# Strassen's seven products for the first matmul of a second MLP layer, over pairs of token chunks, on one Trainium2 core

## The chip, the cores and the metric

The kernel runs on one core of one Trainium2 chip. The metric is the device time of one execution in microseconds (us), median of three. Engines: PE (TensorE), DVE (VectorE), ACT (ScalarE), POOL (GpSimd) and SP, whose queue issues all the DMAs.

## What is computed

Attention over pooled keys and values, and two MLP layers behind it, all in float32:

```python
q, k, v: [8, 8, 576, 64]      # pool = 8, Sp = 72
k_p = k.reshape(B, H, Sp, pool, D).mean(axis=3)
v_p = v.reshape(B, H, Sp, pool, D).mean(axis=3)
scores = scale * np.matmul(q, k_p.transpose(0, 1, 3, 2))
...                            # softmax, times v_p
x = np.ascontiguousarray(attn_out.transpose(0, 2, 1, 3)).reshape(B * S, H * D)   # [4608, 512]
h = np.maximum(x @ w_in, 0.0)         # layer 1, w_in [512, 2048]
y = h * h @ w_out                     # w_out [2048, 512]
h = y @ w_in2                         # layer 2, same shapes
g = np.where(h >= 1, h, np.where(h <= -1, 0.0, (h + 1) ** 2 / 4.0))
out = g @ w_out2
```

## The kernel before

The 4608 tokens are cut into NC = 9 chunks of 512. Layer 1 takes chunks 0 to 8, layer 2 chunks 9 to 17 (c counts through, so NC = 9 is the first chunk of layer 2). d_ff = 2048 is cut into NF = 16 blocks f of 128, d_model = 512 into four blocks.

Every float32 product is made of three fp32r matmuls, on the high and the low part of each operand: high x high, high x low, low x high. `w_hi` and `w_lo` hold both parts of w_in (columns 0 to 511 of each block) and w_out (columns 512 to 1023).

A chunk on PE (`chunk`, L990): for every f, `output(c, f)` (L967; four columns m of the output, three matmuls each, into the four banks of `ps_y`, L985) and then `hidden(f + 2)` (L936; four k blocks by three matmuls into bank f % 2 of `ps_h`, L944), for the last two f of the next chunk. Each is 12 matmuls of 128x128 by 128x512.

Between them an activation makes `g_hl`, two buffers of g's high and low part. Layer 1 (`hidden1`): ACT's relu (L574) and square (L576), DVE's square (L734) and low part (L738). Layer 2 (`hidden2`): DVE clips h (L745), ACT squares (L581), DVE takes the maximum with h (L748), ACT casts the high part (L584), DVE subtracts for the low part (L751).

At a chunk's end layer 1 splits the output once more (`take_y`: ACT L592, DVE L758) and stores both parts to DRAM (`store_y`, L343), from where `load_y` (L313) fetches them as layer 2's operand. Layer 2 copies its output (`take_out`, DVE L765) and stores it (`store_out`, L350). A column of `ps_y` is free for the next chunk once it is taken (`y_taken`).

All queues are written out by hand and served in order: `chunk` on ACT and DVE has the order of the activations, the attention slots of the next batch (chunks 0 to 7 only) and, in chunk NC - 1, the splits of layer 2's weights (L510, L663). SP in the chunks about the change: `store_y(NC-3)`, four `load_x` (L305) for chunk NC - 1, `store_y(NC-2)`, the loads of layer 2's weights, `store_y(NC-1)`, then four `load_y` and a `store_out` for each chunk of layer 2.

## Time and profile before

| | |
|---|---|
| median of 3 runs | 1763.51 us (1763.29 to 1766.1) |
| the profiled execution's own time | 1764.07 us |
| its span, first to last instruction | 1762.3 us |
| PE busy | 1747.7 us (99%) |
| DVE, ACT, POOL busy | 760.3, 552.0, 226.6 us |
| mean granted clock of PE | 0.999 |

PE's busy time counts modelled ends of overlapping matmuls, so it says that PE hardly ever stands still, not that it does the least work it could. Starts of instructions are a sounder measure of its pace than durations. The slices of the page are 44 us each; layer 2 takes the last 18 of the 40.

### The profile page before, as it was taken

What the parts mean: (1) busy time and instruction counts of PE and PEld (TensorE: products, weight loads), DVE (VectorE), ACT (ScalarE), POOL (GpSimd) and SP (SyncE); (2) the same over time, 40 slices, a digit from 0 to 9 for tenths busy, and PEclk for the clock granted to TensorE, in tenths of its full rate; (3) what the DMA queues carried; (4) which work ended last, traced back from release to release, by engine and by line L of the source; (5) the groups of instructions that cost most, each with busy time, mean ns of one, the idle gap of its engine ahead of it and who ended that gap; (6) DMA issues with size and microseconds to landing.
All of it is one profiled execution on the core that took longest, in us unless ns stands there. A gap on an engine that the chain in (4) does not pass through costs nothing.

```text
span 1762.3 us, 22444 instructions
## 1 busy us (share of the span) xinstructions
PE 1747.7 (99%) x8374; PEld 1411.7 (80%) x8374; DVE 760.3 (43%) x1207; ACT 552.0 (31%) x973; POOL 226.6 (13%) x254
## 2 busy tenths in 40 slices
PE   9999999999999999999999999999999999999999
PEld 7777777777777777778888788888888888888887
DVE  6654434444343444443235434343434343434343
ACT  5443333333333333332234322222222222222222
POOL 5422313133131331310000000000000000000000
PEclk9999999999999999999999999999999999999999
DMA  6544233142421424222044202020202020202000
GB/s 167 142 134 130 75 117 86 55 132 74 129 73 61 125 74 132 78 66 96 0 138 149 96 0 72 1 71 0 71 0 71 0 71 0 71 0 71 0 25 24
DMA packets 117072, 126.95 MB, mean 72 GB/s; under 512 B 40192, under 2 KB 72448, under 8 KB 116992
## 3 DMA queue, kind: packets, MB, share of 16 engines
q1 hardware_dynamic: 116992, 125.86, 23.2%
q8 instruction: 53, 0.87, 0.2%
q14 instruction: 27, 0.22, 0.0%
HBM read 80.74 MB, written 45.09 MB: 71 GB/s over the span
## 4 chain that ended last, share of the span: by engine, by line
PE 97%; DVE 2%; issue 0%; ACT 0%; POOL 0%; ACTq 0%; POOLq 0%
PE ps_h L944 44%; PE ps_y L985 44%; PE ps_a L894 2%; PE ps_a L918 2%; PE ps_a L931 2%; PE ps_a L908 1%; DVE sq_f L734 1%; PE ps_y L826 0%; PE ps_a L843 0%; DVE probs L674 0%; PE ps_y L864 0%; ACT act_f L574 0%; DVE stat L672 0%; PE ps_y L875 0%; PE ps_h L854 0%
## 5 line engine op out<-in xcount | busy, mean ns | idle before, releaser
L944 PE MATMUL ps_h<-xc,w_hi 128*128 128x512 f32 x2288 | 715.2, 394 | 0.0
L944 PEld LDWEIGHTS ps_h<-xc,w_hi 128*128 128x128 f32 x2288 | 423.0, 188 | 93.6 <-issue 9.2
L944 PE MATMUL ps_h<-xc,w_lo 128*128 128x512 f32 x1144 | 446.8, 391 | 0.2 <-issue 0.2
L985 PE MATMUL ps_y<-w_hi,g_hl 128*128 128x512 f32 x1152 | 379.4, 390 | 3.1 <-DVE stage L758 2.2
L985 PE MATMUL ps_y<-g_hl,w_hi 128*128 128x512 f32 x1152 | 366.2, 399 | 0.4 <-DVE g_hl L738 0.4
L734 DVE TENSOR_TENSOR sq_f<-act_f 128x512 f32<-128x512 f32 x144 | 111.5, 774 | 408.5 <-ACT act_f L574 402.9
L985 PEld LDWEIGHTS ps_y<-w_hi,g_hl 128*128 128x128 f32 x1152 | 216.9, 188 | 49.1 <-DVE stage L758 2.6
L985 PEld LDWEIGHTS ps_y<-g_hl,w_hi 128*128 128x128 f32 x1152 | 209.6, 188 | 56.2 <-issue 16.3
L581 ACT ACTIVATE act_f<-act_f,half_bias 128x512 f32<-128x512 f32 x144 | 104.1, 723 | 480.1 <-DVE act_f L745 480.1
L944 PEld LDWEIGHTS ps_h<-xc,w_lo 128*128 128x128 f32 x1144 | 214.9, 188 | 47.4 <-issue 0.8
L985 PE MATMUL ps_y<-g_hl,w_lo 128*128 128x512 f32 x576 | 225.7, 392 | 0.0
L985 PE MATMUL ps_y<-w_lo,g_hl 128*128 128x512 f32 x576 | 224.8, 390 | 0.0
L745 DVE TENSOR_SCALAR act_f<-ps_h 128x512 f32<-128x512 f32 x144 | 99.5, 691 | 251.9 <-PE ps_h L944 251.9
L574 ACT ACTIVATE act_f<-ps_h 128x512 f32<-128x512 f32 x144 | 86.0, 598 | 361.3 <-PE ps_h L944 360.5
L748 DVE TENSOR_TENSOR act_f<-ps_h,act_f 128x512 f32<-128x512 f32 x144 | 99.6, 691 | 113.8 <-ACT act_f L581 113.8
L751 DVE TENSOR_TENSOR g_hl<-act_f,g_hl 128x512 fp32r<-128x512 f32 x144 | 99.7, 693 | 98.8 <-ACT g_hl L584 98.8
L450 POOL TENSOR_TENSOR kv_raw<-kv_raw 72x512 f32<-72x512 f32 x112 | 120.5, 1076 | 115.8 <-DMA kv_raw<-in_k 111.4
L985 PEld LDWEIGHTS ps_y<-g_hl,w_lo 128*128 128x128 f32 x576 | 108.1, 188 | 24.5
L985 PEld LDWEIGHTS ps_y<-w_lo,g_hl 128*128 128x128 f32 x576 | 108.5, 188 | 22.4
L584 ACT CAST g_hl<-act_f 128x512 fp32r<-128x512 f32 x144 | 89.3, 620 | 109.1 <-DVE act_f L748 109.1
L738 DVE TENSOR_TENSOR g_hl<-sq_f,g_hl 128x512 fp32r<-128x512 f32 x144 | 109.8, 762 | 7.9 <-DVE sq_f L734 2.4
L467 POOL TENSOR_TENSOR probs<-probs,stat 96x432 f32<-96x432 f32 x56 | 53.5, 955 | 386.8 <-DVE stat L689 386.8
(81 smaller groups left out, 931.2 us busy)
## 6 DMA issues: line engine op xcount, KB each, us to landing
mlp_out_hl<-stage SPq DMA_DIRECT2D x36, 512.0 KB, 4.4
xc<-mlp_out_hl SPq DMA_DIRECT2D x36, 512.0 KB, 5.9
xc<-attn_out_hl SPq DMA_DIRECT2D x32, 512.0 KB, 4.0
attn_out_hl<-xo_hl SPq DMA_DIRECT2D x56, 288.0 KB, 2.3
out<-stage SPq DMA_DIRECT2D x36, 256.0 KB, 2.1
stage<-in_moe_w_in SPq DMA_DIRECT2D x32, 256.0 KB, 3.6
stage<-in_moe_w_out SPq DMA_DIRECT2D x32, 256.0 KB, 4.3
kv_raw<-in_k SPq DMA_DIRECT2D x28, 288.0 KB
```

The costliest lines, as they stand in the source:

```text
L450: nc.gpsimd.tensor_tensor(raw[:, :, 0:width], raw[:, :, 0:width], raw[:, :, width:2 * width], ALU.add).then_inc(kv_add, 1)
L467: nc.gpsimd.tensor_tensor(groups(probs[:, u % 2, :]), groups(probs[:, u % 2, :]), row_stat(u % 2, 3), ALU.mult).then_inc(probs_ready, 1)
L574: nc.scalar.activation(act_f[:, f % 2, :], ps_h[:, f % 2, :], ACT.Relu).then_inc(relu_done, 1)
L581: nc.scalar.activation(act_f[:, f % 2, :], act_f[:, f % 2, :], ACT.Square, bias=half_bias[:, 0:1], scale=0.5).then_inc(ramp_done, 1)
L584: nc.scalar.copy(g_hl[:, f % 2, 0, :], act_f[:, f % 2, :]).then_inc(g_hi_done, 1)
L734: nc.vector.tensor_tensor(sq_f[:, f % 2, :], act_f[:, f % 2, :], act_f[:, f % 2, :], ALU.mult).then_inc(square_done, 1)
L738: nc.vector.tensor_tensor(g_hl[:, f % 2, 1, :], sq_f[:, f % 2, :], g_hl[:, f % 2, 0, :].bitcast(F32), ALU.subtract).then_inc(g_ready, 1)
L745: nc.vector.tensor_scalar(act_f[:, f % 2, :], ps_h[:, f % 2, :], 1.0, -1.0, ALU.min, ALU.max).then_inc(clip_done, 1)
L748: nc.vector.tensor_tensor(act_f[:, f % 2, :], ps_h[:, f % 2, :], act_f[:, f % 2, :], ALU.max).then_inc(bend_done, 1)
L751: nc.vector.tensor_tensor(g_hl[:, f % 2, 1, :], act_f[:, f % 2, :], g_hl[:, f % 2, 0, :].bitcast(F32), ALU.subtract).then_inc(g_ready, 1)
L944: mm = nc.tensor.matmul(ps_h[:, f % 2, :], left[:, f, kd * P:(kd + 1) * P], xc[:, buf, right, kd, :], start=(kd == 0 and n == 0), stop=(kd ...
L985: mm = nc.tensor.matmul(ps_y[:, m, :], left, right, start=(f == 0 and n == 0), stop=(f == NF - 1 and n == 2))
```

## The change

Layer 2's first product is made for two chunks a and b at once, for chunks 1 to 8 of the nine (pair p is chunks NC+1+2p and NC+2+2p); chunk NC stays as it was. A product of 2 x 2 blocks (tokens of a or b, two halves of d_model, two blocks f) takes 7 products by Strassen's scheme (in Winograd's form), with sums and differences of the operands, where it took 8.

- The sums of w_in and their high and low parts are made once, in chunk NC - 2 (`split_wq` on ACT and DVE, SP's `load_wq` and `store_wq`), stored to DRAM (`wq`, 1.8 MB for each of the 8 block pairs), and fetched in layer 2 one block pair at a time into `xc` (`load_wp`).
- `store_y` stores layer 1's output of chunks 1 to 8 once, in float32, without a split; `take_y` is then ACT's copy alone. `load_raw` fetches a pair's tokens; `diff`, `op_high` and `op_low` make the 7 operands of 2 blocks each in the space of w_in.
- PE, phase a: in step s it makes the outputs of chunk a for blocks 2s and 2s+1, and between their columns the 7 products of block pair s + 1, in the order of `STEP`. The products cycle through four banks, `ps_a` and `ps_h`. The activation's inputs are sums of products, made by DVE (`combine`); ACT adds 1, cuts at 0 and squares (`ramp`), DVE clips and takes the maximum (`bend`). Chunk a's g goes to `g_hl` at once, chunk b's stays on chip in float32 (`g_late`, tile `late(f)`).
- PE, phase b: the outputs of chunk b from `late(f)`, high part by ACT (`g_high`), low part by DVE (`g_low`). Meanwhile ACT and DVE make the next pair's operands (`HIGH_AT`, `LOW_AT`, `DIFF_AT`), and in the last step PE makes the next pair's first 7 products.
- On SP the first two attention chunks are taken out of the loop, as chunk 0's output is still stored in two parts. POOL sets one more constant.

The diff, cut to its core (empty lines left out):

```diff
+    NP = NF // 2
+    NPAIR = (NC - 1) // 2
+    PRODUCTS = [(0, 0), (4, 2), (1, 3), (5, 5), (2, 4), (3, 1), (6, 6)]
...
+    STEP = [(None, 0), (0, 0), (None, 1), (0, 1), (None, 2), (0, 2), (None, 3), (0, 3), (None, 4), (1, 0), (None, 5),
+            (1, 1), (1, 2), (1, 3), (None, 6)]
...
+    DIFF_AT = {4: [(T1, 0), (T1, 1), (T2, 0)], 5: [(T2, 1)], 7: [(T4, 0), (T4, 1)], 8: [(T3, 0), (T3, 1)]}
+    HIGH_AT = {4: SPLITS[0:2], 5: SPLITS[2:5], 6: SPLITS[5:8], 8: SPLITS[8:10], 9: SPLITS[10:12], 10: SPLITS[12:14]}
+    LOW_AT = {5: SPLITS[0:2], 6: SPLITS[2:5], 7: SPLITS[5:6], 8: SPLITS[6:7], 9: SPLITS[7:10], 10: SPLITS[10:13],
+              11: SPLITS[13:14]}
...
+                    if c.at(0):
+                        sp.dma_start(ys_v[m, :, :, bass.ds(c.times(CHUNK), CHUNK)],
+                                     stage[:, m, :].rearrange("p (l t) -> p l t", l=2)
+                                     ).then_inc(y_stored[m], DMA)
+                    else:
+                        sp.dma_start(ys_v[m, :, 0, bass.ds(c.times(CHUNK), CHUNK)], stage[:, m, 0:CHUNK]
+                                     ).then_inc(y_stored[m], DMA)
...
+                if n >= 2:
+                    sp.wait_ge(wq_ready, 3 * (n - 1))
+                sp.dma_start(wq_raw[:, n % 2], w_in2.rearrange("(k p) (f c) -> f p k c", p=P, c=2 * P)[n]
+                             ).then_inc(wq_loaded[n % 2], DMA)
...
+            def load_wp(n):
+                sp.dma_start(pieces(n % 2 * NPROD, NPROD).bitcast(F32), wq[n]).then_inc(wp_loaded[n % 2], DMA)
...
+                for s in range(NP - 2):
+                    sp.wait_ge(product_done, p.times(NP * NPROD, NPROD * (s + 1)))
+                    load_wp(s + 2)
+                if more:
+                    sp.wait_ge(product_done, p.times(NP * NPROD, NPROD * (NP - 1)))
+                    load_wp(0)
+                    sp.wait_ge(product_done, p.times(NP * NPROD, NPROD * NP))
+                    load_raw(False, p.plus(1))
+                store_out(a)
+                if more:
+                    sp.wait_ge(op_ready, p.times(2 * NPROD, 4 * NPROD))
+                    load_wp(1)
+                store_out(a.plus(1))
...
+            load_wq(0)
+            load_wq(1)
+            for n in range(NP):
+                store_wq(n)
+                if n + 2 < NP:
+                    load_wq(n + 2)
...
+            for half in range(2):
+                sp.wait_ge(wq_stored[half], DMA * NP)
+            load_raw(True, At(0))
...
+            sp.wait_ge(h_ready, NC * NF)
+            load_wp(0)
+            sp.wait_ge(h_ready, (NC + 1) * NF)
+            load_wp(1)
+            store_out(At(NC))
+            with sp.Fori(0, NPAIR - 1) as i:
+                pair(At(0, i, 1), At(NC + 1, i, 2), True)
+            pair(At(NPAIR - 1), At(2 * NC - 2), False)
...
+                    if c.at(0):
+                        nc.scalar.copy(stage[:, m, 0:CHUNK].bitcast(F32R), ps_y[:, m, :]).then_inc(y_hi_done, 1)
+                    else:
                         act.wait_ge(y_stored[m], c.times(DMA))
-                    nc.scalar.copy(stage[:, m, 0:CHUNK].bitcast(F32R), ps_y[:, m, :]).then_inc(y_hi_done, 1)
+                        nc.scalar.copy(stage[:, m, 0:CHUNK], ps_y[:, m, :]).then_inc(y_taken, 1)
...
+                if part == 0:
+                    act.wait_ge(wq_loaded[n % 2], DMA * (n // 2 + 1))
...
+                    nc.scalar.copy(wq_hl[:, 0:2, 0], wq_raw[:, n % 2, :, 0:P].rearrange("p (o j) c -> p o j c", o=2)
+                                   ).then_inc(wq_hi_done, 1)
+                    nc.scalar.copy(wq_hl[:, 2, 0], wq_raw[:, n % 2, 2:4, P:2 * P]).then_inc(wq_hi_done, 1)
+                else:
+                    act.wait_ge(wq_sum_done, 4 * (n + 1))
...
+                nc.scalar.copy(w_hi[:, n, 0:DM], split_input(first, o, j)).then_inc(op_hi_done, 1)
...
+                act.wait_ge(y_step, c.times(YS, f - 1 if f >= 2 else -YS + NF - 1 if f == 0 else 0))
+                nc.scalar.copy(g_hl[:, f % 2, 0, :], source).then_inc(g_hi_done, 1)
+            def ramp(g, n, tile, h, at):
+                act.wait_ge(sum_ready, g.times(NPROD, at))
+                nc.scalar.activation(tile, h, ACT.Relu, bias=one_bias[:, 0:1]).then_inc(pair_relu, 1)
+                act.wait_ge(pair_relu, g.times(4, n))
+                nc.scalar.activation(tile, tile, ACT.Square, scale=0.5).then_inc(pair_ramp, 1)
...
+            def pair_step(a, g, fp):
+                act.wait_ge(product_done, g.times(NPROD, 1))
...
+                nc.scalar.copy(p1_copy, pair_bank[NPROD * fp % 4]).then_inc(p1_copied, 1)
+                ramp(g, 1, act_f[:, 0, :], p1_copy, 2)
+                act.wait_ge(pair_bend, g.times(4, 1))
+                g_high(a, 2 * fp, act_f[:, 0, :])
+                ramp(g, 2, act_f[:, 1, :], h21, 4)
+                ramp(g, 3, late(2 * fp + 1), u3, 5)
+                act.wait_ge(pair_bend, g.times(4, 2))
+                g_high(a, 2 * fp + 1, act_f[:, 1, :])
+                ramp(g, 4, late(2 * fp), u2, 7)
+            def pair(p, a, more):
+                b = a.plus(1)
+                for s in range(NP - 1):
+                    pair_step(a, p.times_at(NP, s + 1), s + 1)
+                for f in range(NF):
+                    act.wait_ge(pair_bend, p.times(4 * NP, 4 * (f // 2 + 1)))
+                    g_high(b, f, late(f))
+                    if more:
+                        for o, j in HIGH_AT.get(f, []):
+                            op_high(False, p.plus(1), o, j)
+                if more:
...
+                    if c.at(NC - 2):
+                        split_wq(f // 2, f % 2)
+                    if c.at(NC):
+                        for o, j in HIGH_AT.get(f - 2, []):
...
+            def split_wq(n, part):
...
+                if part == 0:
...
+                    nc.vector.tensor_tensor(wq_sum[:, 0], a21, a22, ALU.add).then_inc(wq_sum_done, 1)
+                    nc.vector.tensor_tensor(wq_sum[:, 2], a11, a21, ALU.subtract).then_inc(wq_sum_done, 1)
...
+                    nc.vector.tensor_tensor(wq_sum[:, 1], wq_sum[:, 0], a11, ALU.subtract).then_inc(wq_sum_done, 1)
...
+                    nc.vector.tensor_tensor(wq_sum[:, 3], a12, wq_sum[:, 1], ALU.subtract).then_inc(wq_sum_done, 1)
+                else:
...
+                nc.vector.tensor_tensor(diff_tile[o, j], left, right, ALU.subtract).then_inc(diff_done, 1)
...
+                nc.vector.tensor_tensor(w_lo[:, n, 0:DM], split_input(first, o, j), w_hi[:, n, 0:DM].bitcast(F32),
...
+            def g_low(c, f, source):
...
+                nc.vector.tensor_tensor(g_hl[:, f % 2, 1, :], source, g_hl[:, f % 2, 0, :].bitcast(F32),
...
+            def bend(g, n, tile, h):
...
+                nc.vector.scalar_tensor_tensor(tile, tile, 1.0, h, ALU.min, ALU.max).then_inc(pair_bend, 1)
...
+                dve.wait_ge(p1_copied, g.times(1, 1))
...
+                combine(1, u2, p6, p1_copy)
+                dve.wait_ge(sum_ready, g.times(NPROD, 1))
+                combine(2, p1_copy, p2, p1_copy)
+                combine(3, u3, p7, u2)
+                bend(g, 1, t11, p1_copy)
+                g_low(a, 2 * fp, t11)
+                dve.wait_ge(sum_ready, g.times(NPROD, 3))
+                combine(4, h21, u3, p4, ALU.subtract)
+                dve.wait_ge(sum_ready, g.times(NPROD, 4))
+                combine(5, u3, p5, u3)
+                combine(5, u2, p5, u2)
+                bend(g, 2, t21, h21)
+                bend(g, 3, t22, u3)
+                if taking is not None:
+                    take_out(taking)
+                g_low(a, 2 * fp + 1, t21)
+                dve.wait_ge(sum_ready, g.times(NPROD, 6))
+                combine(6, u2, p3, u2)
+                bend(g, 4, t12, u2)
...
+                for f in range(NF):
+                    g_low(b, f, late(f))
+                    if f == 0:
+                        take_out(a)
+                    if more:
+                        pair_ops(False, p.plus(1), f)
+                if more:
+                    pair_step(b.plus(1), p.times_at(NP, NP), 0, b)
+                else:
+                    take_out(b)
...
+                    if c.at(NC - 2):
+                        split_wq(f // 2, f % 2)
+                    if c.at(NC):
+                        pair_ops(True, At(0), f - 2)
...
+            pair_step(At(NC + 1), At(0), 0, At(NC))
...
-                for m in range(MT):
+                if 0 in columns:
+                    pe.wait_ge(g_ready, c.times(NF, f + 1))
+                for m in columns:
...
+            def product(p, g, fp, n):
...
+                if n == 0:
+                    pe.wait_ge(wp_loaded[fp % 2], p.times(DMA * NP // 2, DMA * (fp // 2 + 1)))
+                    if fp == 0:
+                        pe.wait_ge(op_ready, p.times(2 * NPROD, 2 * NPROD))
+                if n < 4 and not g.at(0):
+                    pe.wait_ge(sum_ready, g.times(NPROD, (3, 4, 6, 7)[n] - NPROD))
+                if n == 3 and g.at(0):
+                    pe.wait_ge(g_ready, (NC + 1) * NF)
+                if n == 4:
+                    pe.wait_ge(p1_copied, g.times(1, 1))
+                if n > 4:
+                    pe.wait_ge(sum_ready, g.times(NPROD, n - 4))
+                weights = piece(fp % 2 * NPROD + left)
+                for j in range(2):
+                    hi, lo = weights[:, j * P:(j + 1) * P], weights[:, (2 + j) * P:(3 + j) * P]
+                    for i, (lhs, rhs) in enumerate(((hi, w_hi), (hi, w_lo), (lo, w_hi))):
+                        mm = nc.tensor.matmul(bank, lhs, rhs[:, 2 * right + j, 0:DM],
+                                              start=(j == 0 and i == 0),
+                                              stop=(j == 1 and i == 2))
+                mm.then_inc(product_done, 1)
+            def pair_step(c, f, p=None, g=None, fp=None):
+                for of, n in STEP:
+                    if of is not None:
+                        output(c, f + of, 2, [n])
+                    elif g is not None:
+                        product(p, g, fp, n)
...
+                for s in range(NP):
+                    if s + 1 < NP:
+                        pair_step(a, 2 * s, p, p.times_at(NP, s + 1), s + 1)
+                    else:
+                        pair_step(a, 2 * s)
+                for s in range(NP):
+                    if s + 1 == NP and more:
+                        pair_step(b, 2 * s, p.plus(1), p.times_at(NP, NP), 0)
+                    else:
+                        pair_step(b, 2 * s)
...
+                for f in range(NF if layer == 1 else NF - 2):
...
+            chunk(At(NC), 1, False, 2)
+            pair_step(At(NC), NF - 2, At(0), At(0), 0)
+            with pe.Fori(0, NPAIR - 1) as i:
+                pair(At(0, i, 1), At(NC + 1, i, 2), True)
+            pair(At(NPAIR - 1), At(2 * NC - 2), False)
```

## Rows read from the trace of the kernel before

**Rows 1.** The page: busy time by engine, and the granted clock in 40 slices.

```profile
PE 1747.7 (99%) x8374; PEld 1411.7 (80%) x8374; DVE 760.3 (43%) x1207; ACT 552.0 (31%) x973; POOL 226.6 (13%) x254
...
PEclk9999999999999999999999999999999999999999
```

**Rows 2.** The page: the chain that ended last, by engine.

```profile
PE 97%; DVE 2%; issue 0%; ACT 0%; POOL 0%; ACTq 0%; POOLq 0%
```

**Rows 3.** PE's waits from 800 to 1762 us: in total, times, longest.

```profile
PE ps_y L985 <- DVE stage L758: 2.2, 1, 2.2
PE ps_y L985 <- DVE g_hl L751: 0.9, 1, 0.9
```

**Rows 4.** Timeline of PE: start, length (us), operation, [idle before].

```profile
1202.72 0.39 PE L985 MATMUL ps_y<-w_hi,g_hl 128*128 128x512 f32 x1
...
1205.44 0.61 PE L944 MATMUL ps_h<-xc,w_hi 128*128 128x512 f32 x2
```

**Rows 5.** Timeline of DVE: one block's chain, and the next clip.

```profile
1202.92 0.69 DVE L745 TENSOR_SCALAR act_f<-ps_h 128x512 f32<-128x512 f32 x1 [1.89 <-PE ps_h L944]
...
1205.77 0.69 DVE L751 TENSOR_TENSOR g_hl<-act_f,g_hl 128x512 fp32r<-128x512 f32 x1 [0.69 <-ACT g_hl L584]
1208.36 0.69 DVE L745 TENSOR_SCALAR act_f<-ps_h 128x512 f32<-128x512 f32 x1 [1.89 <-PE ps_h L944]
```

**Rows 6.** Groups by line: count, busy us, mean ns, idle before with releasers.

```profile
L581 ACT ACTIVATE act_f<-act_f,half_bias 128x512 f32<-128x512 f32 x144 | 104.1, 723 | 480.1 <-DVE act_f L745 480.1
...
L584 ACT CAST g_hl<-act_f 128x512 fp32r<-128x512 f32 x144 | 89.3, 620 | 109.1 <-DVE act_f L748 109.1
...
L748 DVE TENSOR_TENSOR act_f<-ps_h,act_f 128x512 f32<-128x512 f32 x144 | 99.6, 691 | 113.8 <-ACT act_f L581 113.8
...
L734 DVE TENSOR_TENSOR sq_f<-act_f 128x512 f32<-128x512 f32 x144 | 111.5, 774 | 408.5 <-ACT act_f L574 402.9 <-issue 5.6
...
L679 DVE TENSOR_TENSOR xo_hl<-ps_a,xo_hl 128x288 fp32r<-128x288 f32 x56 | 25.2, 451 | 32.4 <-ACT xo_hl L565 32.4
...
L674 DVE TENSOR_TENSOR probs<-ps_a,stat 96x432 f32<-96x432 f32 x56 | 33.8, 603 | 1.9
```

**Rows 7.** Timeline where a layer-2 chunk begins: first output block, the copies.

```profile
1153.76 0.39 PE L985 MATMUL ps_y<-w_hi,g_hl 128*128 128x512 f32 x1
...
1156.48 0.61 PE L944 MATMUL ps_h<-xc,w_hi 128*128 128x512 f32 x2
...
1151.98 2.48 DVE L765 COPY stage<-ps_y 128x512 f32<-128x512 f32 x4
```

**Rows 8.** L985's instructions: what its idle time waited for, us and times.

```profile
  issue: 16.3, 37
```

**Rows 9.** Start of chunk NC - 2: SP's issues, PE's first output; windows.

```profile
798.99 3.09 SPq L343 DMA_DIRECT2D mlp_out_hl<-stage  x4
802.20 3.70 SPq L305 DMA_DIRECT2D xc<-attn_out_hl  x4
...
801.54 0.62 PE L985 MATMUL ps_y<-g_hl,w_hi 128*128 128x512 f32 x2
...
800.00:812.00 12.00, 12.00 (x55) 9.94 (x54) 3.52 (x6) 2.46 (x4) 0.00 (x0) 1.00 0.99 345
896.00:902.00 6.00, 6.00 (x28) 4.95 (x28) 1.67 (x3) 1.23 (x2) 0.00 (x0) 1.00 0.93 291
```

**Rows 10.** Layer 2's start: timeline, and a window (us, busy by engine, PEclk, DMA share, GB/s).

```profile
976.58 2.06 ACT L592 CAST stage<-ps_y 128x512 fp32r<-128x512 f32 x4 [1.47 <-DVE w_lo L663]
...
977.95 0.19 PEld L985 LDWEIGHTS ps_y<-w_hi,g_hl 128*128 128x128 f32 x1 [2.59 <-DVE stage L758]
...
981.99 0.59 PEld L944 LDWEIGHTS ps_h<-xc,w_hi 128*128 128x128 f32 x2
...
980.00:982.00 2.00, 2.00 (x7) 1.52 (x6) 0.97 (x2) 0.93 (x2) 0.00 (x0) 0.50 1.03 381
```

**Rows 11.** Timeline at the tail: the last output block.

```profile
1755.96 0.50 PE L985 MATMUL ps_y<-w_hi,g_hl 128*128 128x512 f32 x1 [0.93 <-DVE g_hl L751]
```

204 lines of the change are left out of this document (166 added, 38 removed).

## The prediction

> **What bounds the kernel now.** The page comes first: TensorE (PE) is busy 99% of the span, VectorE 43%, ScalarE 31%, and the granted clock reads 9 in every slice [rows 1]. The chain of waits gives PE 97% of the span [rows 2]. The list of waits, cut to the part after attention, then shows how little PE lacks: it waits twice, 2.2 us for layer 2's first output columns and 0.9 us for the last block of g [rows 3]. So time is the number of TensorE slots times the slot, and the question is whether the slots taken out stay out.
>
> The slot is read from two starts on the timeline: the 12 matmuls of an output block run from 1202.72 to 1205.44 [rows 4], 2.72 us, 0.227 us each. The same block's clip starts 5.44 us apart [rows 5], which is 24 slots. The printed matmul durations (0.39) overlap and are of no use for this.
>
> **What the change removes.** Per pair of chunks and per pair of blocks f, the first product took 2 x 2 x 12 = 48 matmuls; now it takes 7 products of 2 (j) x 3 (hi/lo passes) = 42. With 8 block pairs and 4 chunk pairs that is 6 x 32 = 192 slots. The output matmuls stay as they were. 192 x 0.2267 = 43.5 us. The new matmuls have the same operand shapes as the old, so I give them the same slot.
>
> **Phase a (chunk a, products of the next block pair).** A step has 42 + 24 = 66 slots, 14.96 us. In STEP, the products end at 1.36, 3.40, 5.44, 7.48, 9.52, 11.56 and 14.96, an output column (0.68 us) between them. Durations: ScalarE's activation 0.72 [rows 6], which I give both halves of a ramp, a cast 0.62 [rows 6]; VectorE's add or subtract 0.69 [rows 6], and from 0.69 to 0.77 for scalar_tensor_tensor, which the trace doesn't have (L734, the dearest of this size, is 0.77); I take 0.69, as L748 is the nearest form. A dependent instruction on VectorE starts 0.03 later (1.9 us over 56 of L674). VectorE has 7 sums, 4 bends and 2 splits: 13 x 0.72 = 9.4 us of 14.96. ScalarE has 1 copy, 8 ramp halves and 2 casts: 7.6 us. Both fit.
> Then order. Both engines are served in order, so I walk the step; a bank can be read 0.2 us after its last slot's end, as the clip at 1202.92 follows the block that ends at 1202.72 [rows 4, 5]. Third sum at 7.7, first bend 9.1, g of the even block ready at 10.5, wanted by PE at 16.3 (next step, after product 0). Fourth sum 11.2, both fifth sums 13.1, bends to 14.8, odd block's g 15.5, wanted at 24.5. Last sum 16.2, last bend 18.4; the next step's first sum wants that tile free at 18.6. The banks come free at 7.7 (wanted 14.96), 11.2 (17.0), 13.1 (19.0), 16.2 (21.1); the copy of product 0 is made by 18.3 (23.1). The smallest PE slack is some 5 us. Where chunk b of the last pair is taken out in the same step, VectorE has four copies more, 2.48 us [rows 7]: the last sum moves to 18.8 (21.1), still 2.3 us in hand. I charge nothing; without this cover each us costs 1 us in each of 32 steps.
>
> **More waits.** Some 10 waits stand in a step of 66 slots. The row for this is the chunk boundary: the output block with four column waits runs from 1153.76 to 1156.48 [rows 7], 2.72 us again, so a met wait costs nothing. From above, the trace books 16.3 us of idle on 37 weight loads of L985 [rows 8]: 0.44 each over 320 waits is 141 us, and 0.14 each eats the gain. The boundary is the nearer case: 0.
>
> **From a to b.** Formerly a block of the first product covered take_out; now output(b, 0) follows output(a, 15). With output(a, 15) ending at 5.44 after the last step, the column copies (0.60 apart) end at 5.0, 5.7, 6.4, 7.1; they are wanted at 5.44, 6.12, 6.80, 7.48. The next g is ready at 7.8, wanted at 8.16. That is 0.4 us in hand: 0, at most 4 x 1 us.
>
> **Phase b (chunk b's outputs from g kept on chip).** PE takes 2.72 us a block, and between blocks 4 and 11 VectorE has 8 splits of g and 22 operations for the next pair, up to four a block. Back to back (0.60 apart, as the four copies) 2.4 us; each dependent on the one before, 2.9. g's chain (cast, then split: 1.4 us after output f-2) leaves 1.2 us in hand, and 7 blocks x 0.2 = 1.3 uses it up: 0 to 0.3 us at each of three places. I take 0.5 in all; the upper bound is below. Chunk NC carries the same 22 operations inside the old scheme: the chain takes 3.54 us (1202.92 to 1206.46), leaving 1.89 idle [rows 5], and three operations at 0.60 take 1.8. Here g is ready 1.7 us before PE wants it (1206.46; its output block starts 5.44 after 1202.72, at 1208.16): nothing.
>
> **Transfers.** A step needs 1.8 MB of weight sums. The engines moved 345 GB/s over 12 us [rows 9], so 5.3 us of 14.96, issued a whole step ahead. Storing the sums in chunk NC-2 moves 2.3 MB in 10.9 us (two blocks), 215 GB/s. Hidden. load_y in layer 2 goes, load_raw (2.1 MB a pair) comes in behind the last products, 6.1 us at that rate, with one block pair and four blocks, 16 us, to its first use. In layer 1 store_y shrinks, and VectorE loses 2.48 us a chunk that PE never waited for [rows 3]: 0.
> One transfer is not: the first two-block piece of w_in. SP queues it behind store_y of NC-3 and four load_x. Before, those are issued at 798.99 and 802.20 and fill the engines until 812 [rows 9]. Now store_y is half as large and, ScalarE alone freeing it, 0.9 us earlier: 3.15 MB from 799.1 at 345 GB/s end at 808.2; 0.52 MB more at the 291 GB/s of narrower rows 1.8 us, a little for the landing: 810.5. ScalarE and VectorE both stand at split_wq(0, 0), ahead of hidden1(2) in their queues. Then copies 1.0, relu 0.6, square 0.7, split 0.7 (the four sums of 256 columns, 0.45 each at most [rows 6], lie beside): g(2) at 813.6 to 814. PE wants it two double blocks after 801.54, at 812.42. Stall 1.5 us; bounds 0 and 5. Then g(3) is ready 1.8 us early.
>
> **What comes back.** take_y is now one copy on ScalarE. At chunk NC-1's end PE idles until the first column is split; ScalarE's first copy is done at 977.1 [rows 10], 0.8 us before PE restarts at 977.95. That idle also brings the granted clock down to 0.50, the 1.2 GHz level: 12 weight loads from 977.95 to 981.99 take 4.04 us for 2.72, and 1.5 us are lost with the few after. Idle of 0.9 us at the tail [rows 11] leaves the clock alone. Idle of 1.4 and 1.5 us, here and at the w_in piece, lies between; I count half the 1.5 at each. So this boundary gives 0.8 + 0.7 = 1.5 back, and the piece costs 1.5 + 0.7 = 2.2. The tail stall goes, since the last blocks' g lies ready: 1.1 us (0.93 and the overlap).
>
> **A rule that speaks against it.** The rows show the products' predecessor already alternating between a ps_h and a ps_y bank every 12 matmuls with the clock at 9 tenths or more [rows 1, 4]. The Trainium skill, "TensorE: Matmul & The Clock Gate", section "A second HAM failure mode: psum-queue depth-cycling", says that cycling through PSUM banks with micro-idles between groups made the clock fall and rise again and again. By the trace the sum keeps 43.5 us; by that rule it would be rival 4, about 1960, as the new steps cycle through four banks and change group every 3 or 6 matmuls.
>
> **Sum.** 1764.07 (the profiled execution) - 43.5 - 1.5 - 1.1 + 2.2 + 0.5 = 1720.7. The execution lies 0.56 above the median of 1763.51, so 1720.
>
> **Rivals.**
> 1. VectorE bounds phase b. At 0.77 + 0.03 an operation four take 3.2 us for 2.72; 0.5 x 8 blocks x 3 = 12 us: 1732. For it: the tightest place. Against: SBUF operations of layer 2 run at 0.69.
> 2. The w_in piece is late by the full 5 us and the clock falls: 6.5 for 2.2, 1724 to 1725.
> 3. The in-order chain in phase a is longer than walked, so that PE waits about 1 us a step: 32 us, 1752. It needs over 2 us more than my walk has.
> 4. Slower: TensorE falls to 1.2 GHz in the steps with products. A slot there is twice 0.227. The gain is gone once 192 extra slots are lost, 87 us spent at the low level out of 32 x 15 = 480. Half the steps' slots at that level cost 1056 x 0.227 = 240 us: about 1960. Against it: the clock fell in the rows only after 2.2 us of idle.
> 5. The slots don't go, or come at a longer interval (0.24 for 0.227 over 2112 + 1500 slots is all of the gain): no change, 1763.
>
> **How the numbers follow.** Forecast (1715 to 1724) 0.68; rival 1 with partial cases 0.09; rival 2 0.09; rival 3 0.07; rival 4 0.04; rival 5 0.03. Without both clock halves and w_in stall the sum is 1716; rivals 1 and 2 end at 1732. So 1714 to 1733 holds a little over 8 in 10. Within 0.2% (3.5 us, what a measurement of this kernel tells from nothing): 0.02; slower 0.04; faster 0.94.
>
> **What would show it.** L985 with the new product line: 192 fewer matmuls; steps of 14.96 us in phase a, 43.5 us per 16 output blocks in b; PE idle at 812 of 1 to 2 us for a g_hl split; at the NC boundary 1.4 for 2.2; the tail wait gone; clock slices at 9 throughout. Wrong if products wait for sums in each step, if g in blocks 5 to 11 of phase b is late, or if the clock falls in layer 2.

## The result, and the profile after

| | before | changed |
|---|---|---|
| median of 4 runs each | 1764.44 us (1763.29 to 1766.1) | 1717.05 us (1716.59 to 1717.49) |
| ratio to before, 95% interval | | 0.9739 [0.9727, 0.975] |
| profiled execution: time; span | 1764.07; 1762.3 | 1716.59; 1714.8 |
| mean granted clock | | 1.0 |

The change makes the kernel 2.6% faster. The profiled spans differ by 47.5 us, 4.0 more than the 43.5 us of the slots taken out, and that 4.0 is itself a sum of parts with both signs, which the rest of this text takes apart.

The page of the changed kernel, the lines that answer to [rows 1, 2], and one group of DMA issues (operation, count, KB each, us from issue to landing):

```profile
PE 1701.4 (99%) x8182; PEld 1374.1 (80%) x8182; DVE 871.0 (51%) x1415; ACT 688.8 (40%) x1213; POOL 229.2 (13%) x255
...
PE 95%; DVE 2%; issue 1%; ACT 1%; DMA 1%; SPq 0%; POOL 0%; DVEq 0%; ACTq 0%; POOLq 0%
...
xc<-w_in_ops SPq DMA_DIRECT2D x32, 1792.0 KB, 7.2
```

PE has 192 matmuls fewer (8374 to 8182) and is still the bound; its granted clock reads 9 in every slice. VectorE went from 43% to 51% and ScalarE from 31% to 40%, and neither became the bound. The loads of weight sums land 7.2 us after their issue, half of a 15 us step. In the chain PE has 95% where it had 97%: the new entry "DMA" is the wait for the w_in piece, and 10.9 us of "issue" are what VectorE does ahead of L1317; both come below.

The list of PE's waits over the whole span, without the 1.0 us at the start (in total, times, longest; the answer to [rows 3]; the waits on `probs` lie in attention, ahead of the window of [rows 3]):

```profile
PE ps_a L1237 <- DVE probs L872: 3.4, 7, 1.5
PE ps_y L1292 <- DVE g_hl L936: 1.9, 2, 1.5
PE ps_a L1317 <- DVE sq_f L1021: 1.9, 2, 1.0
PE ps_y L1292 <- ACT stage L721: 1.5, 1, 1.5
```

L1317 is the new product line, L1292 the output matmuls. The output line waits once for `stage` (start of layer 2, 1.5 us for 2.2) and twice for `g_hl`: 1.5 us at the w_in piece, and 0.4 us in the first 60 us of the program, where the kernel before has the same wait. The tail's 0.9 us is gone. The waits on `probs` are 3.4 us in all for 6.5 before; experiments 8 and 11 show why. What no step of the prediction had is the third line: L1317 waits twice, 1.0 us each, for a sum of VectorE.

Where they lie, on PE's timeline (start, length, operation, idle before with its releaser), with three starts of an ordinary step of phase a:

```profile
808.71 0.73 PE L1292 MATMUL ps_y<-g_hl,w_hi 128*128 128x512 f32 x2 [1.49 <-DVE g_hl L936]
...
973.74 0.47 PE L1292 MATMUL ps_y<-w_hi,g_hl 128*128 128x512 f32 x1 [1.53 <-ACT stage L721]
...
1069.02 0.39 PE L1317 MATMUL ps_a<-w_hi,xc 128*128 128x512 f32 x1
...
1070.38 0.39 PE L1292 MATMUL ps_y<-w_hi,g_hl 128*128 128x512 f32 x1
...
1071.06 0.39 PE L1317 MATMUL ps_h<-w_hi,xc 128*128 128x512 f32 x1
...
1239.47 0.50 PE L1317 MATMUL ps_a<-w_hi,xc 128*128 128x512 f32 x1 [0.97 <-DVE sq_f L1021]
...
1404.07 0.50 PE L1317 MATMUL ps_a<-w_hi,xc 128*128 128x512 f32 x1 [0.96 <-DVE sq_f L1021]
```

From 1069.02 to 1070.38 are the six matmuls of one product (1.36 us), from there to 1071.06 an output column of three (0.68): 0.227 us a slot, as before, with a change of bank and several met waits between them. Layer 2's matmuls run from 973.74 to 1711.3, 737.6 us. 3240 slots at 0.2267 are 734.5; the other 3.1 us go with the two waits at L1317 (experiment 1).

The clock at the start of layer 2 (us, busy by engine, PEclk, DMA share, GB/s), the answer to the window of [rows 10]:

```profile
973.00:980.00 7.00, 6.26 (x28) 5.23 (x29) 2.50 (x4) 3.29 (x6) 0.00 (x0) 1.00 0.83 293
```

It stays at 1.00, the 2.4 GHz level, after 1.5 us of idle. In [rows 10] it fell to 0.50 after 2.2.

**Layer 1.** The prediction charged its changes nothing. The start of each chunk can be marked by ScalarE's first copy out of ps_y (one such copy stands in [rows 10]). Three such marks of the kernel before, then of the changed one:

```profile
253.97 2.14 ACT L592 CAST stage<-ps_y 128x512 fp32r<-128x512 f32 x4
...
362.24 2.14 ACT L592 CAST stage<-ps_y 128x512 fp32r<-128x512 f32 x4
...
471.34 2.14 ACT L592 CAST stage<-ps_y 128x512 fp32r<-128x512 f32 x4
```

```profile
253.25 2.14 ACT L721 COPY stage<-ps_y 128x512 f32<-128x512 f32 x4
...
360.98 2.14 ACT L721 COPY stage<-ps_y 128x512 f32<-128x512 f32 x4
...
468.71 2.14 ACT L721 COPY stage<-ps_y 128x512 f32<-128x512 f32 x4
```

Chunks of 108.27 and 109.10 us before are 107.73 and 107.73 now. All marks, as differences: before 108.34, 108.27, 109.10, 108.27, 109.60, 108.26; after 107.75, 107.73, 107.73, 107.74, 107.96, 107.70. Each chunk is some 0.55 us shorter, and two of them, the third and the fifth, had 0.8 and 1.3 more on top. At chunk NC - 2 the changed kernel is 5.4 us ahead. So there are two things to explain that the prediction did not have: 5.4 us gained where nothing was expected, and some 3 us lost in layer 2.

### The profile page after: what moved, and what is told of

Its sections match the earlier page's. It is cut to its first block, busy times and chain, and to the rows that moved or that the text cites. A ratio compares the mean times of both kernels' runs of the same rounds, so it can differ in the third digit from the quotient of the medians.

```text
span 1714.8 us, 23006 instructions
## 1 busy us (share of the span) xinstructions
PE 1701.4 (99%) x8182; PEld 1374.1 (80%) x8182; DVE 871.0 (51%) x1415; ACT 688.8 (40%) x1213; POOL 229.2 (13%) x255
## 4 chain that ended last, share of the span: by engine, by line
PE 95%; DVE 2%; issue 1%; ACT 1%; DMA 1%; SPq 0%; POOL 0%; DVEq 0%; ACTq 0%; POOLq 0%
PE ps_y L1292 44%; PE ps_h L1250 25%; PE ps_a L1317 9%; PE ps_h L1317 8%; PE ps_a L1200 2%; PE ps_a L1224 2%; PE ps_a L1237 2%; PE ps_a L1214 1%; DMA wq_raw<-in_moe_w_in 1%; PE ps_y L1132 0%; DVE sq_f L932 0%; PE ps_a L1149 0%; DVE probs L872 0%; PE ps_y L1170 0%; ACT act_f L701 0%
## 5 line engine op out<-in xcount | busy, mean ns | idle before, releaser
L1250 PE MATMUL ps_h<-xc,w_hi 128*128 128x512 f32 x1264 | 399.2, 397 | 0.0
L1292 PE MATMUL ps_y<-w_hi,g_hl 128*128 128x512 f32 x1152 | 388.9, 389 | 1.5 <-ACT stage L721 1.5
L1292 PE MATMUL ps_y<-g_hl,w_hi 128*128 128x512 f32 x1152 | 365.6, 398 | 1.9 <-DVE g_hl L936 1.9
L1250 PEld LDWEIGHTS ps_h<-xc,w_hi 128*128 128x128 f32 x1264 | 230.7, 188 | 52.9 <-issue 9.2
L1292 PEld LDWEIGHTS ps_y<-g_hl,w_hi 128*128 128x128 f32 x1152 | 209.6, 188 | 57.3 <-issue 16.5
L1292 PEld LDWEIGHTS ps_y<-w_hi,g_hl 128*128 128x128 f32 x1152 | 216.2, 188 | 46.9 <-DVE w_lo L861 1.9
L1250 PE MATMUL ps_h<-xc,w_lo 128*128 128x512 f32 x632 | 247.3, 391 | 0.0
L1292 PE MATMUL ps_y<-g_hl,w_lo 128*128 128x512 f32 x576 | 225.3, 391 | 0.0
L1292 PE MATMUL ps_y<-w_lo,g_hl 128*128 128x512 f32 x576 | 224.1, 389 | 0.0
L1317 PE MATMUL ps_a<-w_hi,xc 128*128 128x512 f32 x448 | 155.3, 390 | 2.0 <-DVE sq_f L1021 1.9
L1317 PE MATMUL ps_h<-w_hi,xc 128*128 128x512 f32 x448 | 154.8, 389 | 0.0
L1250 PEld LDWEIGHTS ps_h<-xc,w_lo 128*128 128x128 f32 x632 | 118.6, 188 | 26.2
L1292 PEld LDWEIGHTS ps_y<-g_hl,w_lo 128*128 128x128 f32 x576 | 108.1, 188 | 24.0
L1292 PEld LDWEIGHTS ps_y<-w_lo,g_hl 128*128 128x128 f32 x576 | 108.1, 188 | 22.4
L1317 PEld LDWEIGHTS ps_a<-w_hi,xc 128*128 128x128 f32 x448 | 84.1, 188 | 20.9 <-DVE sq_f L1021 3.5
L1317 PEld LDWEIGHTS ps_h<-w_hi,xc 128*128 128x128 f32 x448 | 84.1, 188 | 17.5
L703 ACT ACTIVATE g_hl<-act_f 128x512 fp32r<-128x512 f32 x144 | 91.1, 633 | 4.6
```

The costliest lines, as they stand in the source:

```text
L703: nc.scalar.activation(g_hl[:, f % 2, 0, :], act_f[:, f % 2, :], ACT.Square).then_inc(g_hi_done, 1)
L1250: mm = nc.tensor.matmul(ps_h[:, f % 2, :], left[:, f, kd * P:(kd + 1) * P], xc[:, buf, right, kd, :], start=(kd == 0 and n == 0), stop=(kd ...
L1292: mm = nc.tensor.matmul(ps_y[:, m, :], left, right, start=(f == 0 and n == 0), stop=(f == NF - 1 and n == 2))
L1317: mm = nc.tensor.matmul(bank, lhs, rhs[:, 2 * right + j, 0:DM], start=(j == 0 and i == 0), stop=(j == 1 and i == 2))
```

## What VectorE does at the wait of L1317

VectorE's timeline of the changed kernel around the first of these waits, and the pieces of the chain of waits between (start, us, what), then windows of the same stretch:

```profile
1232.83 0.69 DVE L1014 SCALAR_TENSOR_TENSOR g_late<-g_late,sq_f 128x512 f32<-128x512 f32 x1 [1.46 <-ACT g_late L757]
...
1238.72 0.69 DVE L1021 TENSOR_TENSOR sq_f<-ps_a,sq_f 128x512 f32<-128x512 f32 x1 [5.20 <-PE ps_h L1317]
```

```profile
1232.92 0.06 DVEq L1123
1232.97 5.45 issue
1238.42 0.06 DVEq L1123
```

```profile
1232.00:1234.00 2.00, 2.00 (x10) 1.69 (x9) 0.69 (x1) 1.24 (x3) 0.00 (x0) 1.00 1.13 323
...
1236.00:1238.00 2.00, 2.00 (x11) 1.65 (x10) 0.00 (x0) 0.00 (x0) 0.00 (x0) 1.00 0.65 269
```

VectorE stands still for 5.2 us. The first line names PE as the releaser, but the chain books the same time as "issue" between two entries of L1123, and L1123 is no sum: it is the loop `with dve.Fori(0, NPAIR - 1) as i:` over the pairs of chunks. The pause is the jump from the loop's end back to its start. It comes at the ends of the first two pairs; the third pair stands outside the loop and has none. From 1232 to 1238 the DMA engines move 269 to 358 GB/s (the stores of the pair before and the first load of the next sums). The 5.2 us eat the slack of phase a, and PE lacks some 1.5 us at each of the two (0.97 and 0.96 of it in the waits).

The view of the DMA queues shows what is fetched then. Cut to 0.1 us from 1236.50 it has, beside the data's queue, a packet of a queue of kind "instruction" (packets, MB, share of 16 engines' time):

```profile
q14 instruction: 1, 0.01, 19.3%
```

From 1228 to 1244 there are three such packets, at 1236.5, 1239.0 and 1241.4. The first comes 3.5 us after the jump at 1232.97, and VectorE goes on 1.9 us after it, at 1238.42. That q14 is VectorE's queue, and what the time before its first packet consists of, the experiments show.

## The experiments

Each ran beside the kernel before. A ratio is to that, with its 95% interval.

**1. The jump itself.** The pair loop of VectorE alone is written out, so that it never jumps; the transfers stay.

```diff
-            with dve.Fori(0, NPAIR - 1) as i:
-                pair(At(0, i, 1), At(NC + 1, i, 2), True)
+            for i in range(NPAIR - 1):
+                pair(At(i), At(NC + 1 + 2 * i), True)
```

> In the changed kernel VectorE stands still for 5.2 us (1233.52 to 1238.72) right where its loop over pairs jumps back, and TensorE then waits 1.4 us for a sum; the same at 1403. Here VectorE's loop over pairs is written out, and nothing else is changed. If the stall is the jump back, both waits go: TensorE's waits on L1021 are 0 and the span is 2.8 us shorter, 1712.0. If the stall comes from the two transfers that land at that time (or from my walk being too short by itself), it stays with code in a straight line: 1714.8.

Measured: 1713.09 us (1713.03 to 1715.32), 0.9721 [0.9708, 0.9734], span 1711.3. PE's list of waits has no L1317 left; the other lines stand as they were (`probs` 3.5 for 3.4). Layer 2's matmuls, from the first start to the last end, take 734.5 us for 737.6, which is what 3240 slots come to: the two jumps cost PE 3.1 us, and the same transfers without the jump cost nothing. Of the rest of the 3.5 us of the span, 1.2 were gained ahead of layer 2, where the two kernels have the same work (0.5 of them by the first chunk's mark, 144.95 for 145.50), and 0.8 were lost behind the last matmul. Its page has 7 packets of instructions fewer (the changed kernel's line ahead, this one's behind), and from 1228 to 1244 none:

```profile
q14 instruction: 34, 0.28, 0.1%
```

```profile
q14 instruction: 27, 0.22, 0.0%
```

q14 is VectorE's, and the pair loop's jumps are what it fetched for.

**2. The transfers beside it.** The first load of the sums for the next pair waits for three products more, so that the engines are idle at the jump.

```diff
-                    sp.wait_ge(product_done, p.times(NP * NPROD, NPROD * (s + 1)))
+                    sp.wait_ge(product_done, p.times(NP * NPROD, NPROD * (s + 1) + (3 if s == 0 else 0)))
                     load_wp(s + 2)
```

> VectorE's loop stays, but the 1.8 MB load that SP issues just when VectorE jumps back (1231.18) is issued three products later. Theory: after the jump VectorE's instructions come by DMA and stand behind that load (engines busy until about 1237.5, VectorE resumes 1238.4). Then its pause falls from 5.2 to 2 us or less, TensorE's waits there go, and the span is about 1712. Rival: the pause is a fixed cost of the jump; then it stays 5.2 and the span 1714.8. The load still lands before block pair 2 needs it (7.2 us, issued 9.5 us ahead).

Measured: 1715.94 us (1715.65 to 1716.74), 0.9732 [0.9718, 0.9745], span 1714.7: no gain where one was expected. Layer 2's matmuls take 738.2 us for 737.6. The reading is in VectorE's timeline, the chain's "issue" pieces, and SP's issue of the delayed load:

```profile
1235.60 0.69 DVE L1021 TENSOR_TENSOR sq_f<-ps_a,sq_f 128x512 f32<-128x512 f32 x1 [2.77 <-PE ps_h L1317]
1241.32 0.69 DVE L1021 TENSOR_TENSOR sq_f<-ps_a,sq_f 128x512 f32<-128x512 f32 x1 [5.03 <-issue]
```

```profile
1232.28 3.02 issue
...
1236.29 4.86 issue
```

```profile
1233.08 11.00 SPq L441 DMA_DIRECT2D xc<-w_in_ops  x2
```

With the engines idle for the first 0.8 us the jump takes 3.0 us. One sum is done, and then VectorE stands again, for 4.9 us, under the load issued at 1233.08. The view of the queues has a q14 packet in the 0.1 us from 1233.50 and one in the 0.1 us from 1239.40. The first comes 1.2 us after the jump at 1232.28, for 3.5 in the changed kernel; the second 5.9 us after the first, for 2.5. After each VectorE starts within 1.8 to 1.9 us (1235.36, 1241.18), as in the changed kernel. So where a jump back fetches, it costs about 3.0 us with hardly any transfer beside it, the instructions come in pieces, and a piece whose packet meets a load arrives 2 to 3 us later. The delayed load only moved that delay from the first piece to the second: PE's L1317 waits fall to 1.0 in all, and a new wait for `g_hl` takes 1.0. Neither theory was right alone.

**3. The copies out of PSUM in layer 1.** VectorE's half of take_y is put back for layer 1, with the small stores of the changed kernel.

```diff
-                        nc.scalar.copy(stage[:, m, 0:CHUNK], ps_y[:, m, :]).then_inc(y_taken, 1)
+                        nc.scalar.copy(stage[:, m, 0:CHUNK], ps_y[:, m, :]).then_inc(y_hi_done, 1)
...
-                        if c.at(0):
+                        if layer == 1:
                             take_y(c)
```

> VectorE's half of take_y is put back for layer 1's chunks 1 to 8 (four subtractions, 2.5 us, ahead of its next work, and the column is free only after them); the stores stay half as large. The changed kernel reached chunk 7 5.4 us earlier than the kernel before, which my prediction had at 0. If these subtractions were the cause, layer 1 loses most of it again: 1718 to 1720. If the smaller stores were the cause, it stays near 1714.8 (plus 0.8 at the start of layer 2).

Measured: 1717.1 us (1715.98 to 1720.4), 0.974 [0.9727, 0.9754], span 1714.9. The chunks of layer 1 stay at 107.63 (one with a jump 108.40). The theory that VectorE's 2.48 us cost PE something in every chunk falls. Its `stage` wait at layer 2's start is back at 2.3 us (1.5 in the changed kernel), which shows the prediction's 0.8 there, and with it the granted clock is at the 1.2 GHz level again (0.50 from 975.5 to 978.5); the w_in piece waits 2.4 for 1.5.

That the span is nevertheless that of the changed kernel has a reason in the jumps. VectorE's queue over one pass of the loop in layer 1, from 366 to 582 us, first in the changed kernel, then here; and VectorE's first sums behind the jump of the pair loop here, the line that answers to the one with 5.20 above:

```profile
q14 instruction: 1, 0.01, 0.0%
```

```profile
q14 instruction: 6, 0.05, 0.1%
```

```profile
1236.86 1.51 DVE L1021 TENSOR_TENSOR sq_f<-ps_a,sq_f 128x512 f32<-128x512 f32 x2
```

In the changed kernel VectorE's loop in layer 1 jumps back within 0.4 us, and no packet comes; with the four subtractions a chunk put back, packets come at 367.4 and 583.5, and the jumps take 3.6 and 3.5 us. At the pair loop, whose code is the same in both kernels, it is the other way round: 5.2 us of idle and three packets in the changed kernel, 0.4 us and no packet here, and PE waits for no sum at L1317. Layer 2's matmuls take 736.1 us: 3240 slots and the 1.6 of the clock. So a jump back costs something only where it fetches, and an edit elsewhere in the engine's queue decides whether it does.

**4. The same with the full stores.** As 3, and chunks 1 to 7 store both halves again.

```diff
-                    if c.at(0):
+                    if not c.at(NC - 1):
                         sp.dma_start(ys_v[m, :, :, bass
```

> As the run with VectorE's half put back, and the stores of chunks 1 to 7 are again 512 KB a column. Theory: the transfers, not the subtractions, make VectorE's jump back in layer 1 long (5.6 and 5.2 us at 369 and 586 in the kernel before, under 4.4 in the changed one); then this run loses another 1.5 to 2.5 us, at the starts of chunks 3 and 5 only, and is 5.4 to 6 us over 1714.8 in all. Rival: the store size does nothing, and it equals the run before it.

Measured: 1724.07 us (1722.91 to 1724.8), 0.9775 [0.9762, 0.9789], span 1722.6. Its chunk marks, and PE's longest wait:

```profile
360.16 2.14 ACT L721 COPY stage<-ps_y 128x512 f32<-128x512 f32 x4
...
469.23 2.14 ACT L721 COPY stage<-ps_y 128x512 f32<-128x512 f32 x4
...
576.86 2.14 ACT L721 COPY stage<-ps_y 128x512 f32<-128x512 f32 x4
```

```profile
PE ps_y L1292 <- DVE g_hl L936: 6.1, 2, 5.7
```

The third and the fifth chunk are 109.07, the fourth 107.63. Beside the larger stores the loop's jumps take 5.6 and 5.8 us for 3.6 and 3.5 in experiment 3, and the two chunks are 1.44 longer than the steady one each, for 0.77 and 0: the delay of experiment 2 in another loop. The other chunks are left alone. And the larger stores hold up the first piece of w_in: PE stalls 5.7 us for it, and the granted clock is 0.50 from 814 to 820. This makes the run 7.8 us longer than the changed kernel, for 5.4 to 6 expected. The shorter steady chunk comes from neither the copies nor the stores.

**5. Are the slots worth what they were priced at?** One product of the seven (n == 6) is computed twice, with no more waits, so the 48 slots are back.

```diff
-                for j in range(2):
+                for j in (0, 1, 0, 1) if n == 6 else (0, 1):
```

> The last product of each step is computed twice (its six matmuls run again and give the same result), so the number of TensorE slots is that of the kernel before, with all else as in the changed one. If the change's gain is the 192 slots at 0.2267 us, this is 43.5 us slower than the changed kernel: span 1758.3. If a part of the product's time was cover for waits on VectorE and ScalarE, the extra slots absorb those 2.8 us and it is 1755.5. If the gain came from elsewhere (layer 1, boundaries), it is far less than 40 us slower.

Measured: 1765.82 us (1762.77 to 1767.13, 10 runs), 1.0012 [1.0003, 1.0022], span 1764.4. That is 49.6 us more than the changed kernel, not 43.5. The rest stands in PE's waits, its timeline at the first, and a window behind it:

```profile
PE ps_h L1317 <- issue: 5.4, 2, 2.8
```

```profile
1244.44 0.39 PE L1317 MATMUL ps_h<-w_hi,xc 128*128 128x512 f32 x1 [2.82 <-issue]
```

```profile
1244.00:1248.00 4.00, 3.56 (x10) 2.79 (x10) 0.69 (x1) 0.63 (x2) 0.00 (x0) 0.61 0.89 335
```

PE's own jump back of the pair loop, invisible in the changed kernel, now stops it for 2.8 us, twice, while the engines move 314 GB/s (1241.6 to 1244.4); and the granted clock falls to the 1.2 GHz level behind each (0.61 over the window). The view of the queues has a packet of another instruction queue in the 0.1 us from 1241.60, where PE stopped:

```profile
q8 instruction: 1, 0.02, 74.1%
```

In the changed kernel this queue has none from 1228 to 1244; over the whole program it has 77 packets here and 59 there. The 3.1 us that VectorE's jumps cost PE are gone, as the longer products give it slack. 43.5 - 3.1 + 5.4 leaves 3.8 of the 49.6; 0.4 of them lie ahead of layer 2, and 3.4 are the two falls of the clock. Slots and pauses were mixed here, so experiment 10 repeats this without jumps.

**6. The first w_in piece ahead of the store.** In SP's queue the two loads are issued before the store of chunk NC - 3.

```diff
+            for par in range(2):
+                sp.wait_ge(x_stored[par], x_count(At(B), par, 0))
+            load_wq(0)
+            load_wq(1)
             store_y(At(NC - 3))
```

> SP issues the first two pieces of w_in ahead of chunk NC-3's stores and of the four loads of x. By my account of the 1.5 to 1.9 us stall at 808 (VectorE and ScalarE stand at the piece that is queued behind 3.1 MB) it goes: span 1712.9, no wait of TensorE on g_hl there. If the stall comes from the extra work itself (copies and sums ahead of the activation, 1.0 to 1.6 us), at least 1 us of it stays.

Measured: 1714.78 us (1713.61 to 1717.48), 0.9728 [0.9715, 0.9741], span 1713.0. The stall at the piece is gone (the `g_hl` line falls from 1.9, 2 times, to the 0.5 at the program's start), and the chunk takes 87.98 for 89.76: the piece had cost 1.8. The waits at the jumps of layer 2 grew from 1.9 to 2.8 in all: their length is not the same from one program to the next.

**7. The boundary of the layers.** The last take of layer 1 goes into tiles of `g_late` that are free by then, and the last weight split moves behind the next activation.

```diff
+                    elif c.at(NC - 1):
...
+                        nc.scalar.copy(g_late[:, 8 + m, :], ps_y[:, m, :]).then_inc(y_taken, 1)
...
-                        if c.at(NC - 1):
-                            split_w(2 * NF - 1)
-                            act.wait_ge(w_ready, 2 * NF - 3)
                         take_y(c)
```

> At the end of layer 1 the last chunk's output is taken into four free tiles of g_late instead of the stage that still holds weights, the last weight split moves behind the next activation, and TensorE's wait for all splits before chunk NC is left out (each block's own wait stays). If the stall at 973 (1.5 us, 1.9 with the weight loads) is that chain of splits, it goes: 1712.9. If output columns would come too late anyway, some stays. If the later split makes g(1) or the stores late, a new wait appears on g_hl in chunk NC.

Measured: 1715.45 us (1714.59 to 1718.38), 0.9732 [0.9719, 0.9746], span 1714.1. The `stage` wait of 1.5 us is gone. The span is 0.7 shorter for 1.9 expected, as the waits at the jumps are 3.0 for 1.9.

**8. Did the kernel before lose time at its jumps?** In the kernel before, VectorE's loop over the attention chunks is written out.

```diff
-            with dve.Fori(0, (NC - 3) // 2) as i:
-                chunk(At(1, i, 2), True, 1)
-                chunk(At(2, i, 2), True, 1)
+            for c in range(1, NC - 2):
+                chunk(At(c), True, 1)
```

> The kernel before, with VectorE's loop over the attention chunks written out. It idles 5.6 and 5.2 us at the jumps back (369 and 586), and chunks 3 and 5 take 0.8 and 1.3 us more than chunks 1, 2, 4 and 6. If the jump is the cause, those 2.1 us go: 1.6 to 2.1 us faster, 1762.0 for 1764.07. If the long chunks have another cause, no change.

Measured: 1760.59 us (1759.78 to 1764.99, 11 runs), 0.999 [0.9981, 0.9999], span 1758.0 for 1762.3. The chunks are 108.28, 108.26, 108.29, 108.27, 108.26, 108.30: the 0.8 and 1.3 of the third and fifth are gone, and the rest is as it was. q14 has 20 packets for 27. PE's idle at the start of layer 2 is 2.2 us again, yet in this execution the window behind it shows no fall of the clock:

```profile
976.00:982.00 6.00, 6.00 (x28) 4.96 (x28) 3.65 (x6) 1.61 (x3) 0.00 (x0) 1.00 1.00 341
```

From its first copy out of ps_y at layer 2's start to the end it is 1.6 us shorter than the kernel before: that much of the 4.3 us is the clock. So 2.2 us of idle does not bring the fall each time, but by the mean clock mostly it does. Of the 48 executions of the kernel before that ran beside these experiments 41 have a mean granted clock of 0.999, as the profiled one with its fall, and 7 have 1.0, the five fastest of all among them. Of the 11 here 7 have 1.0.

**9. All the remedies together.** The changed kernel with VectorE's two loops written out (edits 1 and 8) and edits 6 and 7.

> The changed kernel with VectorE's loops over chunks and over pairs written out, the first pieces of w_in ahead of the other transfers, and the last take of layer 1 aside. If the three waits of TensorE that these removed one by one are independent, the span is 1714.8 - 3.5 - 1.9 - 1.9 = 1707.5. In the runs with one of the last two alone, the waits at VectorE's jump back grew by about 1 us; if that was the jump, it cannot happen here.

Measured: 1709.88 us (1709.45 to 1710.02), 0.9692 [0.9678, 0.9705], span 1708.2. It beats both kernels, and its span is 0.7 us over the expected sum. PE's list of waits is down to 3.5 on `probs` in attention, 1.0 at the start and 0.5 for `g_hl`; the latter is the wait at the program's start, which the 1.9 taken for the w_in piece had in it.

**10. The eighth product without jumps.** Edit 5, with the pair loops of PE and VectorE written out. To be held against experiment 1.

> The run with the last product computed twice was 49.6 us longer instead of 43.5: TensorE stood twice for 2.8 and 2.6 us with nothing that it waited for, and the granted clock fell after each. Here TensorE's and VectorE's loops over pairs are written out too. If these were TensorE's own jumps back, they go, and the span is 43.5 us over that of the changed kernel with VectorE's loop written out (1711.3): 1754.8. If they come from the longer steps, the span stays near 1761 to 1764.

Measured: 1759.44 us (1757.77 to 1760.28, 7 runs), 0.997 [0.9959, 0.9981], span 1757.8, no wait on "issue". From the mark of chunk NC (ScalarE's first copy at the start of layer 2) to the end it takes 783.0 us (974.81 to 1757.8), and the kernel of experiment 1 takes 739.5 (971.82 to 1711.3). The difference is 43.5, the 192 slots at 0.2267. The 3.0 us by which the whole was longer than expected lie ahead of that mark, where the two kernels have the same work; 2.3 of them are there at the first chunk's mark (147.22 for 144.95), in the start of the program. The cause of that is not shown.

**11. Where the tiles lie.** In the kernel before, three small tiles (`half_bias`, one of the size of the new `one_bias`, `warm_exp`) are placed ahead of `q_raw`, so that the tiles of attention lie 12 bytes further, as in the changed kernel. No instruction differs.

```diff
+        half_bias = sb("half_bias", [P, 1])
+        one_bias = sb("one_bias", [P, 1])
+        warm_exp = sb("warm_exp", [P, 1])
         q_raw = sb("q_raw", [QT, 2, NJ, 2, D])
```

> The kernel before with half_bias and warm_exp placed ahead of the attention's tiles, with a third of the same size, as in the changed kernel, so that all of attention's tiles lie 12 bytes further. In the changed kernel each attention chunk took 107.6 to 107.7 us for 108.3, whether take_y and the stores were put back or not. If the place of the tiles is the cause, attention chunks take 107.7 here and the kernel is 3 to 4 us faster; if not, 108.3, and the cause lies elsewhere.

Measured: 1760.64 us (1758.07 to 1762.27, 11 runs), 0.998 [0.9971, 0.9989], span 1760.4. Two marks of it:

```profile
255.35 2.14 ACT L593 CAST stage<-ps_y 128x512 fp32r<-128x512 f32 x4
...
363.11 2.14 ACT L593 CAST stage<-ps_y 128x512 fp32r<-128x512 f32 x4
```

The chunks are 107.71, 107.76, 109.72, 107.68, 108.99, 107.68: the steady chunk is 0.57 shorter, as in the changed kernel, and the jumps still cost 2.0 and 1.3. The profiled span is only 1.9 shorter, as this execution reached its first mark 2.0 us later (147.64 for 145.63); the medians differ by 3.25. The place of the tiles makes the steady difference.

Where in the chunk it lies, the timelines show. The same place of one chunk, in the kernel before and here: POOL's second addition of a pair on `kv_raw`, VectorE's square, and the one wait of PE for `probs` in the chunk:

```profile
271.24 0.74 POOL L450 TENSOR_TENSOR kv_raw<-kv_raw 72x256 f32<-72x256 f32 x1
271.26 1.26 DVE L734 TENSOR_TENSOR sq_f<-act_f 128x512 f32<-128x512 f32 x1 [2.33 <-ACT act_f L574]
274.69 0.66 PE L931 MATMUL ps_a<-ident,probs 96*72 96x96 f32 x6 [0.59 <-DVE probs L674]
```

```profile
272.59 0.69 DVE L735 TENSOR_TENSOR sq_f<-act_f 128x512 f32<-128x512 f32 x1 [2.28 <-ACT act_f L575]
272.61 1.27 POOL L451 TENSOR_TENSOR kv_raw<-kv_raw 72x256 f32<-72x256 f32 x1
275.73 0.66 PE L932 MATMUL ps_a<-ident,probs 96*72 96x96 f32 x6 [0.32 <-DVE probs L675]
```

The two instructions start within 0.03 us of each other, and the second to start takes 0.5 to 0.6 us longer. Before, that is VectorE's square, and the `probs` that PE waits for come 0.3 us later for it; here it is POOL's addition, for which nothing waits. All steady chunks of the kernel before and of experiment 8 have the first order; all of the changed kernel, of experiment 1 and of this run have the second. By the starts of PE's matmuls some 0.3 of the 0.57 us arise at this wait, the rest in steps of less than 0.05 us over the chunk. Why 12 bytes turn the order round, no row shows.

## Why the prediction was right

The forecast was 1720.0 and the time 1717.05. With the terms as measured, in us of the profiled span:

| term | predicted | measured |
|---|---|---|
| 192 slots | -43.5 | -43.5 (experiment 10) |
| layer 1: tiles' place; jumps and start | 0 | -3.3; -2.0 |
| start of layer 2: stall; clock | -0.8; -0.7 | -0.7; -1.6 |
| tail | -1.1 | -1.2 |
| first w_in piece: stall; clock | +1.5; +0.7 | +1.8; 0 |
| phase a: VectorE's jumps back | 0 | +3.1 |
| phase b | +0.5 | 0 |
| sum | -43.4 | -47.4 |

The measured terms leave 0.1 of the 47.5 us between the spans. The forecast is good to 3 us in part by luck: the two terms that it put at nothing, layer 1 with 5.3 us to the good and the jumps with 3.1 us to the bad, cancel for the most part.

**The main term** held to a tenth. The new matmuls have the slot of the old ones, in products of six and columns of three, and the met waits between them cost nothing: the row of the chunk boundary [rows 7] was the right one to take, and the 0.14 and 0.44 read off L985's weight loads [rows 8] was idle beside PE's work.

**The walk of phase a** held for the steps it described. One instruction longer would have been needed: the loop's own jump. That a jump can pause was to be seen before. The kernel before has jumps in its attention loop, whose pause VectorE's timeline gives as "issue", and 5.6 us is more than the 5 us of slack that the walk found:

```profile
374.52 0.69 DVE L734 TENSOR_TENSOR sq_f<-act_f 128x512 f32<-128x512 f32 x1 [5.60 <-issue]
```

That this loop's jump would be such a one could not be read there: VectorE's other loop in the kernel before, over the chunks of layer 2, jumps back in 0.4 us, and so does the pair loop itself in experiment 3. Rival 3 was of this kind but put the loss in each of 32 steps. It came at two, for 3.1 us instead of 32.

**Layer 1 at nothing** is the step that failed. Its reason, that PE never waited for VectorE's copies there, was true for the steady chunk (experiment 3). But without these copies the jumps of VectorE's loop fetch nothing and cost next to nothing (experiments 3 and 8); the halved stores beside them would have made them cheaper even so (experiment 4); and the tiles moved (experiment 11). In the sum of the table these are 5.3 us, more than the whole miss of the sum, 4.0; 3.3 of them belong to no part of the scheme: the kernel before with its tiles moved has them too.

**The w_in piece** came as walked, with all of it some 5 us earlier, since layer 1 was ahead: g ready at 808.7 for 813.6 to 814, wanted at 807.1 for 812.4 (24 slots after the output's start at 801.62), PE idle 1.5 us as forecast, and 1.8 lost in the chunk (experiment 6). The first cast after the load and the last split of g:

```profile
805.77 0.62 ACT L728 CAST wq_hl<-wq_raw 128x512 fp32r<-128x512 f32 x1 [8.12 <-DMA wq_raw<-in_moe_w_in]
...
807.96 0.69 DVE L936 TENSOR_TENSOR g_hl<-sq_f,g_hl 128x512 fp32r<-128x512 f32 x1
```

ScalarE and VectorE both stood at the split of the new piece, ahead of g in their queues, as the prediction said. Rival 2, the full 5 us with a fall of the clock, is what experiment 4 shows with the old stores: 5.7, where experiment 3 has 2.4. That difference is the doing of the smaller store.

**The clock.** Half of 1.5 us was counted at each of two idles of 1.5 us; neither brought a fall, and all four executions of the changed kernel have a mean of 1.0. What could not be read from one execution is that the fall in [rows 10] comes in most executions, but not in all (experiment 8). Without it in the execution before, the difference would have been 45.9.

**Phase b** has no PE wait at all. Four operations at 0.60 fit in 2.72 us, and scalar_tensor_tensor, which no row before had, takes 0.69, as its nearest row said. A group of it (count, busy us, mean ns, idle before):

```profile
L1014 DVE SCALAR_TENSOR_TENSOR act_f<-act_f,sq_f 128x512 f32<-128x512 f32 x32 | 21.9, 686 | 4.7 <-ACT act_f L757 4.7
```

That ends rival 1. **Rival 4** found no support: the mean clock is 1.0 over the whole, while the steps of products cycle through four banks and change bank every 3 or 6 matmuls. The kernel before was nearer to this than the prediction said: its output blocks go through the four banks of ps_y in columns of three matmuls, too. The Trainium skill, "TensorE: Matmul & The Clock Gate", section "A second HAM failure mode: psum-queue depth-cycling", speaks of such cycling with micro-idles between the groups; PE has no idle between the groups here, so this trace neither bears the rule out nor tests it. Rival 5 is refuted by the count and the slot.

What stays open: why 12 bytes of shift change which of VectorE and POOL starts first; why a jump back fetches again in some programs and not in others (VectorE's pair loop in experiment 3 and PE's in the changed kernel do not); and why the waits at the jumps vary between 1.9 and 3.0 us from program to program.

## What to carry to other kernels

Where one engine is busy 99% of the span, slots taken out times the slot length is the gain, if each other engine's queue is walked through a step and has slack: here to a tenth of a microsecond in 43.5. Walk the loop's jump back as one of the instructions of every engine, at the length that a pause at a jump has in the trace under the same transfers. Whether it pauses at all has to be read from the trace of the new program, as an edit elsewhere changed it here. A loop whose slack is under the pause is written out; moving the load beside it by 2 us did not help here (experiment 2). Before a few microseconds of a difference are put down to the change, look at stretches that it did not touch: their length can move by the tiles' addresses alone, and here the start of the program varied by 2 us.

## What the runs showed of the hardware

- An engine's jump back can be a pause: VectorE 3.0 us with the DMA engines idle at first, 5.2 to 5.6 at some 300 GB/s. Packets of a queue of kind "instruction" are in the DMA view at that time, and the engine goes on 1.8 to 1.9 us after one. PE's jump stopped it for 2.8 us at 314 GB/s in the kernel with 6 matmuls a step more, and not in the changed kernel.
- A jump back can also cost 0.4 us and fetch nothing. The same loop code did the one in the changed kernel and the other in experiment 3, whose edit lies elsewhere in VectorE's queue.
- A loop's instructions come in pieces, and a transfer issued between them stops the engine a second time (4.9 us in experiment 2).
- A square of VectorE takes 0.69 us and an addition of POOL 0.74. Where the two start within 0.03 us of each other, the second to start takes 1.26 or 1.27 us. A shift of SBUF tiles by 12 bytes turned their order round and changed a chunk of attention and layer 1 from 108.27 to 107.70 us, with the same instructions.
- The granted clock fell to the 1.2 GHz level after 2.2 us of PE idle in the profiled execution of the kernel before, and by the mean of 0.999 in 41 of 48 others, but not in the profiled one of nearly the same program; after 2.3 us it fell (experiment 3), after 2.8 us both times (experiment 5); after 2.4 us at the w_in piece (experiment 3) and after 1.5 us it did not.
